# Small softmax tiles declared behind the large tiles of a fused attention and two-layer network kernel

## The reference, cut to what matters

```python
# attention: 12288 queries of 128, 768 pooled keys; then two layers of width 2048
kv_pool = kv.reshape(B, H // 4, 4, W // 4, 4, C).mean(axis=(2, 4))
k = v = kv_pool.reshape(B, -1, C) @ w_sr
s = (q @ k.transpose(0, 2, 1)) / sqrt(C)
a = exp(s - s.max(-1, keepdims=True))
x = (a / (a.sum(-1, keepdims=True) + 1e-9)) @ v
h = x @ w_in1
g = where(h >= 1, h, where(h <= -1, 0, (h + 1) ** 2 / 4))
y = g @ w_out1
h = y @ w_in2
g = h / (1 + exp(-1.702 * h))
out = g @ w_out2
```

## Time and profile before

| | |
|---|---|
| median of 3 runs | 1349.64 us (1347.39 to 1350.06) |
| profiled execution | 1347.17 us |
| its span, first to last instruction | 1345.3 us |
| mean granted TensorE clock | 0.987 |
| busy: PE, PEld, DVE, ACT, POOL | 1283.4, 1037.9, 1015.5, 1022.4, 1178.8 us |
| matmuls | 5496 |

### The profile page before, as it was taken

The page is one execution under the profiler, slowest core; times in us unless marked ns, Lnnn a source line. Parts: engine busy times, 40 slices in busy tenths (PEclk is TensorE's granted clock), DMA queues, the critical chain, the costliest instruction groups (busy, mean ns, idle before and its releaser), DMA issues.

```text
span 1345.3 us, 17190 instructions
## 1 busy us (share of the span) xinstructions
PE 1283.4 (95%) x5496; PEld 1037.9 (77%) x5496; DVE 1015.5 (75%) x1165; ACT 1022.4 (76%) x1083; POOL 1178.8 (88%) x481
## 2 busy tenths in 40 slices
PE   4577999999999999999999999999999999999988
PEld 2355888888888888888888888888888888878866
DVE  6888787797787887877877867878878778756433
ACT  3756777887878778788878888787887788786756
POOL 1677999999999999999999999999999999998760
PEclk9878999999999999999999999999999999999999
DMA  9100000000000000000000000000000000000000
GB/s 337 40 16 16 9 32 17 16 31 16 16 19 24 20 16 16 31 16 16 31 16 16 31 16 16 16 19 28 16 16 31 16 17 24 8 17 16 0 9 16
DMA packets 18605, 36.19 MB, mean 27 GB/s; under 512 B 3344, under 2 KB 3472, under 8 KB 18320
## 3 DMA queue, kind: packets, MB, share of 16 engines
q1 hardware_dynamic: 18576, 35.83, 8.1%
HBM read 29.43 MB, written 6.39 MB: 27 GB/s over the span
## 4 chain that ended last, share of the span: by engine, by line
PE 81%; POOL 7%; issue 5%; DVE 4%; DMA 2%; ACT 1%; SPq 0%; POOLq 0%; DVEq 0%; ACTq 0%
PE ps_ring L353 15%; PE ps_ring L355 15%; PE ps_ring L354 15%; PE ps_y L353 12%; PE ps_y L355 12%; PE ps_y L354 11%; POOL g_lo L306 3%; POOL g_lo L313 2%; POOL pt_lo L320 1%; DMA kv_sb<-in_kv_t 1%; DVE s_sb L707 1%; DMA key_max<-max_row 1%; DMA max_row<-max_turned 1%; DVE g_hi L751 1%; DVE g L758 1%
## 5 line engine op out<-in xcount | busy, mean ns | idle before, releaser
L313 POOL TENSOR_TENSOR g_lo<-g,g_hi 128x1024 fp32r<-128x1024 f32 x192 | 524.3, 2731 | 90.0 <-DVE g L758 82.2
L306 POOL TENSOR_TENSOR g_lo<-g,g_hi 128x1024 fp32r<-128x1024 f32 x181 | 437.2, 2415 | 4.1 <-ACT g_hi L577 4.1
L751 DVE SCALAR_TENSOR_TENSOR g_hi<-g,ps_ring 128x1024 fp32r<-128x1024 f32 x192 | 234.1, 1219 | 165.9 <-ACT g L591 159.4
L575 ACT ACTIVATE g<-ps_ring 128x1024 f32<-128x1024 f32 x192 | 197.2, 1027 | 188.7 <-PE ps_ring L355 188.5
L353 PE MATMUL ps_y<-g_hi,w_hi 128*128 128x512 f32 x768 | 307.2, 400 | 23.0 <-POOL g_lo L313 19.2
L355 PE MATMUL ps_y<-g_hi,w_lo 128*128 128x512 f32 x768 | 303.6, 395 | 0.0
L354 PE MATMUL ps_y<-g_lo,w_hi 128*128 128x512 f32 x768 | 300.8, 392 | 0.0
L758 DVE SCALAR_TENSOR_TENSOR g<-g,ps_ring 128x1024 f32<-128x1024 f32 x192 | 233.0, 1214 | 0.0
L584 ACT ACTIVATE g<-ps_ring 128x1024 f32<-128x1024 f32 x192 | 197.9, 1031 | 20.7 <-POOL g_lo L313 12.4
L591 ACT ACTIVATE g<-g 128x1024 f32<-128x1024 f32 x192 | 203.7, 1061 | 5.4
L577 ACT ACTIVATE g_hi<-ps_ring 128x1024 fp32r<-128x1024 f32 x192 | 196.1, 1021 | 5.4 <-PE ps_y L355 5.4
(11 more groups left out here) (69 smaller groups left out, 1743.3 us busy)
## 6 DMA issues: line engine op xcount, KB each, us to landing
kv_sb<-in_kv_t SPq DMA_DIRECT2D x12, 512.0 KB, 8.9
q_sb<-in_q_t SPq DMA_DIRECT2D x24, 256.0 KB, 3.7
key_max<-max_row SPq DMA_DIRECT2D x24, 256.0 KB, 3.4
inv_sum<-inv_row SPq DMA_DIRECT2D x24, 256.0 KB, 3.2
out_t<-y_sb SPq DMA_DIRECT2D x24, 256.0 KB, 3.5
w_raw<-in_moe_w_in SPq DMA_DIRECT2D x2, 1024.0 KB, 17.7
max_row<-max_turned SPq DMA_DIRECT2D x24, 2.0 KB, 1.3
inv_row<-inv_turned SPq DMA_DIRECT2D x24, 2.0 KB, 1.3
```

The lines of the kernel that those rows point to most:

```text
L306: nc.gpsimd.tensor_tensor(g2_lo[:, slot, :], g2[:, slot, :], g2_hi[:, slot, :].bitcast(F32), ALU.subtract).then_inc(g2_lo_done, 1)
L313: nc.gpsimd.tensor_tensor(g1_lo[:, slot, :], g1[:, slot, :], g1_hi[:, slot, :].bitcast(F32), ALU.subtract).then_inc(g1_lo_done, 1)
L575: nc.scalar.activation(g2[:, slot, :], ps_h2(k), ACT.Gelu_apprx_sigmoid).then_inc(g2_done, 1)
L751: nc.vector.scalar_tensor_tensor(out=g1_hi[:, uu % 2, :], in0=g1[:, uu % 2, :], scalar=1.0, in1=ps_h1(k), op0=ALU.min, op1=ALU.max).then_i ...
```

## The change

The nine small tiles are declared behind `y2_sb` instead of between the large ones. No instruction, wait, shape or loop differs; only addresses do.

```diff
         q_lo = sb(ctx, "q_lo", [C, T], F32R)
-        part_max = sb(ctx, "part_max", [P, KC, QB])
-        fold_max = sb(ctx, "fold_max", [P, QUADS, QB])
-        row_max = sb(ctx, "row_max", [SQ, SQ])
-        max_turned = sb(ctx, "max_turned", [SQ, SQ])
         key_max = sb(ctx, "key_max", [P, T])
-        part_sum = sb(ctx, "part_sum", [P, KC, QB])
-        fold_sum = sb(ctx, "fold_sum", [P, QUADS, QB])
-        row_sum = sb(ctx, "row_sum", [SQ, SQ])
-        inv_turned = sb(ctx, "inv_turned", [SQ, SQ])
-        eps = sb(ctx, "eps", [SQ, QB])
         inv_sum = sb(ctx, "inv_sum", [P, T])
...
         y1_lo = sb(ctx, "y1_lo", [C, 2, T], F32R)
         y2_sb = sb(ctx, "y2_sb", [C, T])
+        part_max = sb(ctx, "part_max", [P, KC, QB])
+        fold_max = sb(ctx, "fold_max", [P, QUADS, QB])
+        row_max = sb(ctx, "row_max", [SQ, SQ])
+        max_turned = sb(ctx, "max_turned", [SQ, SQ])
+        part_sum = sb(ctx, "part_sum", [P, KC, QB])
+        fold_sum = sb(ctx, "fold_sum", [P, QUADS, QB])
+        row_sum = sb(ctx, "row_sum", [SQ, SQ])
+        inv_turned = sb(ctx, "inv_turned", [SQ, SQ])
+        eps = sb(ctx, "eps", [SQ, QB])
```

## The result

The changed kernel takes 1335.61 us (median of 4 runs, 1335.25 to 1335.95), the kernel before 1348.52 beside it (1346.97 to 1350.06). The ratio is 0.9904, 95% interval 0.9887 to 0.9921: 12.9 us or 1.0% faster, outside the range forecast. The profiled execution took 1335.95 us, its span 1334.1. The two traces differ by 11.2 us of span; the remaining 1.7 us of the medians are scatter, above all of the kernel before, whose traced execution was one of its quicker ones.

The account below looks back on a forecast made before the run. The prediction took TensorE, the number of matmuls times the distance of their starts, as the bound. All terms were zero (ends -10 and +10 us), giving 1349.2 us, no change, with a range of 1342.5 to 1353.5 us.

Parts of the forecast that it names:

- the faster rival: Place of x and y data costs and is now gone: both fall to 226.7 ns a matmul, 1342.0 us; chance 0.18.
- the term of the data of the inner products: TensorE matmuls reading x and y, 2304 of 5496: new start addresses change nothing, taken as zero.
- The bound fell with it: Bound on the x and y matmul term: at best all reach the chunks' rate, -7.6 us; upwards +7.6 us.
- The argument from: The x_lo pass, median 388 ns, was already at the least duration any row shows, from the supposedly bad place.
- The change doesn't do what it says: Rival: moved tiles land 128 bytes above multiples of 2 KB, so nothing changes, 1349.6 us; chance 0.08.
- Data and weights now collide: Rival: inner-product data and weights at equal residue of 2048 obstruct each other, up to +7.6 us, 1357.2 us; chance 0.12.
- Its mark of 229.9 ns for x: Rate of x matmuls above which the slower rival, data and weights reading SBUF at equal residues, would decide.
- The sentence that priced the whole excess at 33 us: If the excess over the 215.8 ns rule were the place's price, x and y gain 33 us; chance under 0.01.
- The other terms: Making x and y, key_max and inv_sum, DMAs, small tiles: zero each, with bounds such as 0.4 and 2 us.
- with 10 us free in 200: GpSimd's slack in the middle windows, said to allow the faster rival, whose gain there would be 1.1 us.

Follow-up runs that it names:

- y_64: Changed kernel with only y1_hi and y1_lo moved to 64 bytes (mod 256) from the weights; 1345.42 us, ratio 0.9974 to the kernel before.
- x_64: Changed kernel with only x_hi and x_lo at 64 bytes (mod 256) from the weights; 1344.69 us, ratio 0.9977 to the kernel before.
- all_zero2: Changed kernel with an unused 1920-byte tile ahead of w_hi, every large tile at a true multiple of 2048; 1335.56 us, ratio 0.9905 to before.
- all_64: Changed kernel with an unused 64-byte tile ahead of w_hi, every large tile at 192 mod 2048; 1335.57 us, ratio 0.9903 to before.
- x_512: Changed kernel with unused tiles placing x_hi and x_lo 512 bytes off the weights mod 2048, y unmoved; 1335.52 us, ratio 0.9901 to before.
- x_256_y_1024: Changed kernel with unused tiles placing x 256 and y 1024 bytes off the weights; 1335.14 us, ratio 0.9897 to before.
- w_apart: Changed kernel with an unused 128-byte tile between w_lo and g1, all data, k and v 128 bytes from w_hi and w_lo; 1356.27 us, ratio 1.0050.
- xy_back2: Changed kernel with an unused 1856-byte tile ahead of x_sb, returning x and y tiles to their old place mod 2048; 1347.67 us, ratio 0.9996.
- w0_with_x: Changed kernel with x_hi, x_lo and their weights, the first part of w_hi and w_lo, all moved by 64 bytes; 1342.22 us, ratio 0.9954.
- w0_alone: Changed kernel with only the weights of x, the first part of w_hi and w_lo, moved by 64 bytes; 1342.11 us, ratio 0.9954.
- xhi_64: Changed kernel with only x_hi at 64 bytes from the weights, x_lo left in line; 1344.05 us, ratio 0.9971 to before.
- w_64: Changed kernel with an unused 64-byte tile between w_lo and g1, all data, k and v 64 bytes from w_hi and w_lo; 1341.95 us, ratio 0.9958.
- xy_32: Changed kernel with x and y tiles at 32 bytes from the weights, x_sb left in line; 1352.41 us, ratio 1.0030 to before.

## Why the prediction was wrong

*The bound was read rightly.* TensorE's distance of starts set the time, and an edit without any instruction could move the time only through it. The matmuls in 200 us, named as the thing to look at, went to 881 where 877 was the mark of the faster rival.

*The step that failed is the term of the data of the inner products.* It was set to zero by the sentence "If the place mattered, x and y would stand together and apart from the three others." That takes each group's rate for the price of its own place. The runs show that it isn't: y_64 slows the aligned x behind it to 231.3 ns, x_64 leaves y at 226.7 and has g at 230.8, exactly the 230.8 of the earlier trace rows. The g of the kernel before was no sample of an aligned group; it was slowed by x and y ahead of it. Nor was x, at 228.3, a sample of an unaligned one: with y in line ahead of it the same place gives 231.7 (x_64). And the slower groups did not owe their rate to having weights in `w_hi` and `w_lo`, as the prediction had it, since with these weights all of them run at 226.7 in the kernel after. The chunks stand behind twelve aligned matmuls, and they were the one control that gave the rate of the kernel after, 226.7. The term, put at 0, measured -14.9 us in 20 iterations, of which GpSimd's waits gave 3.7 back.

*The bound fell with it.* "All x and y matmuls come to the rate of the chunks" gave -7.6 us. The true term has g in it: 24 x 226.7 = 5.44 us for a step of 5.53, 0.75 us an iteration by the means of the timeline, 14.9 us in 20 iterations, twice the bound. The faster rival had the direction and the final rate right, and its price too small.

*The argument from* `x_lo`, "already at the least that any row shows": a recorded duration isn't the cost of a matmul. Its median went from 388 to 390 ns while the group it belongs to got quicker, and that of `g_hi` fell from 397 to 390 without a change of place.

*The change doesn't do what it says* was true in words and false in its use. True multiples of 2 KB are not reached and not needed: all_zero2, all_64, x_512 and x_256_y_1024 all give the time of the kernel after. What the change does is to set x and y at a multiple of 256 bytes from the weights and from the other data.

*Data and weights now collide* is refuted with its sign turned: equal places mod 256 are the best that were tried, and w_apart shows a distance as the price. Its mark of 229.9 ns for x was a slip besides: 228.3 and the 1.2 of its own sum make 229.5.

*The pages.* "SBUF — State Buffer" of the Trainium skill, section "A bandwidth-pool intuition that's wrong", has contention as a matter of ports and locks alone; nineteen kernels here differ in places only and range from 1335.1 to 1356.3 us, so for TensorE's reads of data and weights the measurement decides against reading it as "places are free". "TensorE: Matmul & The Clock Gate", section "Back-to-back issue gap", has the rule that makes 215.8 ns for 512 columns; the page calls it the gap of an isolated matmul and puts a stream of weight loads and matmuls at about 131 ns. No run here shows either: 226.7 ns is the least that the groups of these kernels come to, for fp32r data with a weight load for each matmul. The sentence that priced the whole excess at 33 us was rightly given no weight.

*The other terms* held: ScalarE's `x_hi` stayed at 632 ns, the DMA of `key_max` at 3.4 us, and xy_back2 shows that moving `key_max`, `inv_sum` and the small tiles brings nothing.

*What is given back* was named in the prediction only as room: GpSimd "with 10 us free in 200". It has 9 free now by the windows, and still stops TensorE once or twice an iteration, where `q_lo` and two slow `g1_lo` fall together or where VectorE has held it up before. The mean share of an engine doesn't tell when it becomes a wait.

*Open.* Why a change of place makes a debt, and why following matmuls pay it. The runs fix its marks: it shows in the aligned groups behind (x_64, y_64), it needs no distance inside a matmul (w0_with_x), the weights' place alone starts it (w0_alone), it is not counted by changes (xhi_64), and at the end of 12 aligned matmuls it is paid, since the chunks take 8.16 us in the kernel before as after. Weight loads run beside the matmuls, 163.3 us of them in 200 us in which TensorE is busy throughout; whether the distance that counts is that to a matmul's own weights or to those being loaded meanwhile, no run here separates in a steady state. That TensorE's reads of data and of weights go through SBUF in stretches of 256 bytes, and lose time while the two streams are out of step, would fit the period; it is argued and not shown, and it doesn't say why 32 bytes cost more (120 ns) than 64 (93) and 128 (87).

## What to carry to other kernels

Where TensorE is the bound, lay all tiles that it reads, data and weights alike, at the same place mod 256 bytes of a partition. Small tiles declared between large ones are what broke this here, and the sum of their sizes can be read off the code. The runs show it for fp32r tiles, 512 columns and a weight load for each matmul, and for nothing else. It was worth 1.0% here, up to 1.5% between the best and the worst layout, with no instruction changed. And don't take the rates of neighbouring groups in one trace as independent samples: a stretch can be slow because of the one ahead of it, so a control must stand behind a stretch of its own kind.

## What the runs showed of the hardware that was not expected

A steady distance of 64 bytes between data and weights costs 2.4 ns a matmul of 512 columns (w_64), one of 128 bytes 5.9 ns (w_apart); mixed places in a step cost 52 ns (w0_with_x) to 120 ns (xy_32) for 24 matmuls. The quick rate, 226.7 ns, is the same at every absolute place tried for the whole set of tiles: 0 (all_zero2), 128 (after) and 192 mod 2048 (all_64).

ScalarE's `y_hi` from PSUM, with equal code, took 599 ns (median) in the kernel before and 621 after:

```profile
L516 ACT ACTIVATE y_hi<-ps_y x24: 591/621/621, 119.1 to 1302.9; 128x512 fp32r<-128x512 f32 x24
```

It is 621 and 619 in all_64 and all_zero2 too, and 600 in x_64, where y is in line and the rest is slower, so it goes with the pace of the rest and not with where y lies. A difference of 20 ns between two such instructions, which the prediction had weighed as a possible sign of the place, isn't one.
